# An mLSTM and two expert layers on one core: an added GpSimd drain, counts from TensorE in the capacity search, and moved waits

## The reference

```
logits = x @ w_gate
for idx in argsort(-logits.flatten()):        # best pairs first
    tok, e = idx // E, idx % E
    if assigned[tok] >= 0 or counts[e] >= cap: continue
    assigned[tok] = e; counts[e] += 1
out[assigned == e] = relu(x[assigned == e] @ w1[e]) @ w2[e]
```

## Time and profile before

| what | value |
|---|---|
| median of 3 runs | 793.84 us (792.9 to 794.62) |
| the profiled execution: its time | 794.07 us |
| the profiled execution: its span | 792.3 us |
| TensorE busy | 742.0 us (94%) |
| VectorE busy | 434.4 us (55%) |
| ScalarE busy | 315.5 us (40%) |
| GpSimd busy | 408.8 us (52%) |
| mean granted TensorE clock | 0.888 of full |

### The profile page before, as it was taken

How to read it: one execution, slowest core, us unless ns; L and a number is a source line. 1 busy time by engine, 2 the same in 40 slices (tenths; PEclk the granted TensorE clock), 3 DMA queues, 4 the chain that set the end, 5 groups by cost and what they waited for, 6 DMA issues and landing times.

```text
span 792.3 us, 21203 instructions
## 1 busy us (share of the span) xinstructions
PE 742.0 (94%) x7388; PEld 647.2 (82%) x7388; DVE 434.4 (55%) x1249; ACT 315.5 (40%) x822; POOL 408.8 (52%) x559
## 2 busy tenths in 40 slices
PE   7999999999998888999999999799999999999993
PEld 3677778777777777999999998489999899899993
DVE  7898887766666673365566765723322323322321
ACT  3566667430000002567667776432332332333330
POOL 4686674600000006877888877336475475475540
PEclk9999999855555556999999999899999999999997
DMA  6676668545922202645456445256767967942320
GB/s 173 196 222 185 196 206 275 171 143 170 308 81 82 82 2 61 208 145 196 122 189 197 134 137 171 70 177 191 221 178 201 264 190 195 251 130 83 95 74 0
DMA packets 64452, 126.24 MB, mean 159 GB/s; under 512 B 14712, under 2 KB 46481, under 8 KB 63603
## 3 DMA queue, kind: packets, MB, share of 16 engines
q1 hardware_dynamic: 44770, 84.19, 34.2%
q0 software_dynamic: 7728, 29.92, 12.7%
q10 hardware_dynamic: 11872, 10.99, 5.1%
HBM read 93.58 MB, written 15.34 MB: 137 GB/s over the span
## 4 chain that ended last, share of the span: by engine, by line
PE 79%; DVE 8%; issue 4%; POOL 2%; ACT 2%; DMA 1%; POOLq 0%; ACTq 0%
PE bank L1678 12%; PE bank L1679 12%; PE bank L1680 12%; PE bank L1637 5%; PE bank L1833 3%; PE bank L1714 3%; PE bank L1717 3%; PE bank L1718 3%; PE bank L1442 3%; PE bank L1613 2%; PE bank L1485 2%; PE bank L1515 2%; PE bank L1809 2%; PE bank L1419 2%; PE bank L1808 2%
## 5 line engine op out<-in xcount | busy, mean ns | idle before, releaser
L1678 PE MATMUL bank<-w_hi,hT_hi 128*128 (+1 forms) x440 | 140.9, 320 | 3.5 <-DVE hT_lo L1256 2.9
L1679 PE MATMUL bank<-w_lo,hT_hi 128*128 (+1 forms) x440 | 136.6, 311 | 0.0
L1680 PE MATMUL bank<-w_hi,hT_lo 128*128 (+1 forms) x440 | 136.5, 310 | 0.0
L858 POOL TENSOR_TENSOR w_lo<-w_raw,w_hi 128x320 fp32r<-128x320 f32 x128 | 109.1, 881 | 35.0 <-DMA w_hi<-w_raw 17.6
L829 POOL DMA_INDIRECT routing_arena<-x_rows,routing_arena x24 | 23.5, 977 | 153.5 <-DVE routing_arena L1244 143.6
L845 POOL TENSOR_TENSOR w_lo<-w_raw,w_hi 128x256 fp32r<-128x256 f32 x124 | 94.0, 791 | 3.7 <-ACT w_hi L608 3.0
L1678 PEld LDWEIGHTS bank<-w_hi,hT_hi 128*128 128x128 f32 x440 | 82.7, 188 | 5.7 <-issue 3.1
L1679 PEld LDWEIGHTS bank<-w_lo,hT_hi 128*128 128x128 f32 x440 | 82.8, 188 | 0.0
L1680 PEld LDWEIGHTS bank<-w_hi,hT_lo 128*128 128x128 f32 x440 | 82.7, 188 | 0.0
L694 ACT ACTIVATE hT_hi<-bank 128x512 fp32r<-128x512 f32 x62 | 33.8, 596 | 96.6 <-PE bank L1833 96.6
L1256 DVE SCALAR_TENSOR_TENSOR hT_lo<-bank,hT_hi 128x384 fp32r<-128x384 f32 x64 | 35.7, 558 | 62.6 <-ACT hT_hi L615 62.6
(11 more groups left out here) (296 smaller groups left out, 1819.5 us busy)
## 6 DMA issues: line engine op xcount, KB each, us to landing
w_raw<-in_moe_w SPq DMA_DIRECT2D x16, 1280.0 KB, 7.0
w_raw<-in_moe_w SPq DMA_DIRECT2D x16, 1024.0 KB, 5.6
turn_arena<-in_moe_w2t SPq DMA_DIRECT2D x12, 768.0 KB, 5.3
w_raw<-in_moe_w SPq DMA_DIRECT2D x32, 256.0 KB, 6.8
w_hi<-w_raw POOLq DMA_DIRECT2D x6, 1280.0 KB, 6.2
w_hi<-w_raw POOLq DMA_DIRECT2D x12, 512.0 KB, 6.9
routing_arena<-x_sorted ACTq DMA_DIRECT2D x31, 160.0 KB, 2.6
mlstm_arena<-in_q SPq DMA_DIRECT2D x32, 120.0 KB
```

Of the source, the lines that this page charges most:

```text
L858: return nc.gpsimd.tensor_tensor(w2_part(w2_lo, n)[:, k, :], w2_raw[:, k, :], w2_part(w2_hi, n)[:, k, :], ALU.subtract)
L1678: T.matmul(dst, a_hi, b_hi, start=first, stop=False)
L1679: T.matmul(dst, a_hi, b_lo, start=False, stop=False)
L1680: return T.matmul(dst, a_lo, b_hi, start=False, stop=last)
```

## The change

It has six parts. GpSimd executes a drain behind the store of block 27, four blocks ahead of the end (`NB2 - 4`). The loads of the gates and of c_head raise two semaphores, so that VectorE's scan waits for two loads; behind the first transposes TensorE makes 7 products of ones in place of 14. In `settle` the sum over blocks and its product are gone: VectorE keeps a copy of the eighth round's counts (`way_count`), marks which of the 16 candidates was taken (`way_is`), TensorE multiplies the two, and the room is the smaller of that and the room before. The first expert's three gathers raise three semaphores and the wait between them is gone. The last expert's first down block waits for each slice by itself. In the second layer the turn of block 1 stands between the high and the low products of `first_up`, ScalarE splits block 1 ahead of its ReLUs, and VectorE waits for the low products before it makes the low part of block 1.

```diff
-            sp.dma_start(head_rows[:, :], t["c_head"]).then_inc(ld_gate, 16)
+            sp.dma_start(head_rows[:, :], t["c_head"]).then_inc(ld_head, 16)
...
-            act.wait_ge(ld_gate, 48)
+            act.wait_ge(ld_head, 16)
...
                 act.wait_ge(dve_made, DVED["first_rows"])
                 next_rows(2, 0)
-                with act.Fori(0, NB2 // 2 - 1) as j:
+                x_hi(1, 1)
+                relu(0)
+                hidden_hi(0)
+                next_rows(3, 1)
+                step(1, 1, True, True)
+                with act.Fori(0, NB2 // 2 - 2) as j:
                     for s in range(2):
-                        step(2 * j + s, s, True, True)
+                        step(2 * j + 2 + s, s, True, True)
...
-                    if e == 0 and b == 2:
-                        pool.wait_ge(landed_a, 16)
                     pool.indirect_dma_start(rows[:, b, 0:KT * 128], None, x_sorted[:, :],
-                                            bass.IndirectOffsetOnAxis(ap=order[:, j:j + 1], axis=0)).then_inc(landed_b if e or b == 1 else landed_a, 16)
+                                            bass.IndirectOffsetOnAxis(ap=order[:, j:j + 1], axis=0)).then_inc(landed_b if e else (landed_a, landed_b, landed_c)[b], 16)
...
                                         tokens[:, b, 0:DM], None, bounds_check=N - 1, oob_is_err=False).then_inc(landed_b, 16)
+                if b == NB2 - 4:
+                    pool.drain()
             pool.wait_ge(landed_b, B_STORED + 16 * NB2)
...
-            dve.wait_ge(ld_gate, 48)
+            dve.wait_ge(ld_gate, 32)
...
+                    if r == ROUNDS - 1:
+                        counted = mark(V.tensor_copy(way_count[:, :], bank[6][0:WAYS, 0:E]))
                     dve.wait_ge(kb_ready, n + 1)
...
-                dve.wait_ge(over_ready, ph + 1)
-                with nc.allow_low_precision("counts up to 24 are exact in bf16"):
-                    V.tensor_reduce(osum_b[:, :], over_b.rearrange("p g e -> p e g"), AX.X, ALU.add).then_inc(osum_ready, 1)
+                need(counted)
+                V.scalar_tensor_tensor(way_is[:, :], theta[0:WAYS, :], threshold[ROUNDS % 2][0:WAYS, 0:1], lane[0:WAYS, 0:1],
+                                       ALU.subtract, ALU.is_equal).then_inc(way_ready, 1)
...
-                link(V.tensor_tensor(room[:, :], room[:, :], count_over, ALU.subtract))
+                link(V.scalar_tensor_tensor(room[:, :], over_room, -1.0, room[:, :], ALU.mult, ALU.min))
...
                 x_lo(0, 0)
+                dve.wait_ge(h_ready, 2 + 1)
                 x_lo(1, 1)
...
-            spin(bank[7], 14)
+            spin(bank[7], 7)
...
                 assign(0, over_b)
-                pe.wait_ge(osum_ready, ph + 1)
-                T.matmul(bank[1][:, 0:E], ones[:, :], osum_b[:, :], start=True, stop=True).then_inc(over_count, 1)
-                side(2)
+                side(1)
+                pe.wait_ge(way_ready, ph + 1)
+                T.matmul(bank[1][:, 0:E], way_is[:, 0:1].to_broadcast([WAYS, 128]), way_count[:, :], start=True, stop=True).then_inc(over_count, 1)
+                side(1)
...
-                    pe.wait_ge(hl3_done, FT * (e + 1) + 2)
+                    if not isinstance(e, int) or e < E - 1:
+                        pe.wait_ge(hl3_done, FT * (e + 1) + 2)
                 pe.wait_ge(yb_done, BPE * e + b + 1)
                 for k in range(FT):
+                    if b == 0 and isinstance(e, int) and e == E - 1:
+                        pe.wait_ge(hl3_done, FT * e + k + 1 + 2)
...
-                pe.wait_ge(x_done, 2)
+                turn(1, 1, 1)
                 for f in range(2):
                     for k in range(2):
                         T.matmul(bank[f][:, :], xT_lo[:, k, 0:128], w1_part(w1_hi, 128, k, f), start=False, stop=False)
...
                 first_up()
-                turn(1, 1, 1)
                 turn_hidden(0)
```

More of the change, by code:

```diff
@@ L275, in build @@
         prev_b = carve(128, [E, G], bf16)
-        osum_b = carve(128, [E], bf16)
+        way_is, way_count = carve(WAYS, [1]), carve(WAYS, [E])
         eye = carve(128, [3, 128], bf16)
@@ L337, in build @@
         ld_const = sem("ld_const")
-        ld_gate = sem("ld_gate")
+        ld_gate, ld_head = sem("ld_gate"), sem("ld_head")
         ld_route = sem("ld_route")
@@ L359, in build @@
         ties_ready, rank_ready = sem("ties_ready"), sem("rank_ready")
-        landed_a, landed_b = sem("landed_a"), sem("landed_b")
+        landed_a, landed_b, landed_c = sem("landed_a"), sem("landed_b"), sem("landed_c")
         raw1_ready, raw2_ready = sem("raw1_ready"), sem("raw2_ready")
@@ L388, in build @@
         NROUTE = 14 * 16
-        A_FIRST, B_FIRST = 32, 16
+        A_FIRST, B_FIRST = 16, 16
         A_SCATTERED = A_FIRST + 16 * G
@@ L1122, in _ @@
             rank = bank[4][:, 0:E * G].rearrange("p (e g) -> p e g", e=E)
-            count_over, tie_total = bank[1][:, 0:E], bank[5][:, 0:E]
+            over_room, tie_total = bank[1][:, 0:E], bank[5][:, 0:E]
             lg = logit_bank[:, 0:G * E].rearrange("p (g e) -> p g e", e=E)
@@ L1180, in search, with settle @@
                         link(V.scalar_tensor_tensor(key_rest[:, :], key_hi[:, :], threshold[r % 2][:, 0:1], half_i[:, 1, :], ALU.subtract, ALU.add))
-                return threshold[(ROUNDS - 1) % 2][:, 0:1]
-            def settle(ph, theta):
+                return threshold[(ROUNDS - 1) % 2][:, 0:1], counted
+            def settle(ph, theta, counted):
                 dve.wait_ge(assigned_ready, 2 * ph + 1)
@@ L1212, in _ @@
                 bits = keys(la[:, :, :] if ph else logit[:, :, :])
-                settle(ph, search(ph, bits))
+                settle(ph, *search(ph, bits))
             link(V.tensor_scalar(rest[:, :], taken[:, :], 0.0, None, ALU.is_equal))
@@ L1686, in first_turn3 @@
                 for b in range(BPE):
-                    pe.wait_ge((landed_a, landed_b, landed_a)[b], (16, B_FIRST, A_FIRST)[b])
+                    pe.wait_ge((landed_a, landed_b, landed_c)[b], 16)
                     for k in range(KT):
```

2 lines of the change are left out of this document (1 added, 1 removed).

## The result

| what | before | after |
|---|---|---|
| median | 793.96 us (792.9 to 794.62, 4 runs) | 781.96 us (780.78 to 783.19, 4 runs) |
| ratio | | 0.985, 95% 0.9827 to 0.9873 |
| profiled execution: time, span | 794.07, 792.3 us | 780.78, 779.0 us |

What follows compares the result with a forecast made beforehand. The chain that ended last was 79% TensorE; GpSimd's exit drain was the largest term. Gains 8.5 + 2.0 + 2.0 + 0.8 + 1.2 + 0.8 = 15.3 us took 794.07 to 778.8, stated as 778.5; range 776 to 788.

Steps and rivals of the forecast that it cites:

- rival 2: The drain works, but another engine or the clock takes back half of the other 6.8 us, giving 782; chance 0.08 more.
- The drain: GpSimd behind block 27's store: price goes by DMAs since the last drain, 0.081 us each; gain 8.5 us.
- Rivals 1 and 4: 1: a drain costs the same whatever is pending, 787.3; 4: added drain returns without the work, counted there; chance 0.16.
- The beginning: First loads and products of ones: dropped wait gives 0.45 us, seven fewer products 1.86; taken as 2.0 us gain.
- half beyond 21 us: Sign at the beginning that the prediction is wrong: TensorE's clock still at its half level after 21 us.
- full by 15 to 18: Sign expected in the profile after: TensorE's clock at its full level by 15 to 18 us.
- rival 3: Half clock at the beginning doesn't end, 11 us on: slower than before, up to 818; chance 0.04.
- The searches: Seven search phases: VectorE's scan starts sooner without the reduction of over-threshold tokens, 0.28 us per phase, 2.0 us gain.
- The gathers: First expert's third gather, without its wait, follows the second 1.28 us later; gain 0.8 us.
- the last expert: First down product: one wait per slice frees 1.4 us, of which ScalarE can use 1.2; gain 1.2 us.
- The first two blocks: Second layer: moving block 1's turn ahead of the low products starts its up product sooner; gain 0.8 us.
- with the same 0.79 of issue: Step for the first two blocks: after the move, block 1's up product starts at 520.55 to 520.85 with 0.79 us of issue.

## Why the prediction was right or wrong

**The time and the side** were right, 781.96 in 776 to 788, though 3.5 above the number said. What came is what rival 2 had said (782): the drain works, and the small gains don't add up. Of 6.8 us forecast for the five other edits the runs give 1.6 to 2.5. That the profiled execution fell by 13.29 is in part luck: 2.2 of it are gains that nobody forecast and that another execution of the same code has only in part.

**The drain**: right in size (8.68, forecast 8.5), in its place and in costing nothing there. The price by the number of DMAs, chosen because two measured drains differed in that alone, is now shown at 3, 12, 16, 30, 48 and 106. Rivals 1 and 4 fall. The fixed part of 0.18 was a misreading: of the 184 ns at the start all but 0.05 pass while GpSimd's last memset ahead of it still runs, and so the exit's drain is 0.30 and not 0.42. The Trainium skill (VectorE: DVE Perf Modes, "The DRAIN you can't avoid") gives the DRAINs of preamble and postamble as a constant of about 12 ns on all five engines. At this exit only SyncE's 13 ns agree; GpSimd's 298 to 8974 do not, nor do ScalarE's 607, VectorE's 591 and TensorE's 1193 in the changed kernel. The first store behind the added drain was late by 2.84 us, and nobody waited for it.

**The beginning** (2.0 forecast, 0.27 and 0.94 in the two executions of the changed kernel, and -0.15 to 1.39 in all eight that have its beginning): no gain is shown at all, since the two executions with an unedited beginning read 0 and 0.79. Two steps failed. "7 x 0.43 = 3.0 us of TensorE" priced the products at the half clock of one execution; at full clock 14 take 3.22 us in all, and the missing 7 are worth 0.4 for VectorE. And "TensorE is busy without a gap, so the shift is carried on" was said of what lay behind the place where the shift is lost. The risk I had named, the clock, was the right one, but it took another course: not that the low clock of 11 us stays, but that with fewer products the clock falls later, at 14.8 to 17.1. That happens in 8 of 8 profiled executions with 7 products and the wait unfilled, in none of 3 with 14 (the drain alone, the 14 restored, the same with the rows held; the half clock in the profile of before lies earlier, at 11), and in neither of the 2 with the wait filled. The Trainium skill (TensorE: Matmul & The Clock Gate, on oscillation) says that waits throttle TensorE anew. The traces agree: a wait of 1.56 to 1.58 us stands ahead of each of the eight, and one of 0.34 or 0.16 where the clock stays full. The half clock ends by itself, at 19.0 to 20.5 in four of the eight and at 21.6 to 21.9 in the other four, the first profile among them. So the sign "half beyond 21 us", by which the prediction called itself wrong, was met, and "full by 15 to 18" was not; rival 3, that it doesn't end, never came. The risk was priced at up to 1.5 us in the bounds and at 0.3 in the sum. Named nowhere was the second bound: the loads of the third pair, which move up too and then share the queues with the first pair's cumulated rows. It binds the kernel before too where its clock is full, so moving VectorE's chain up could not have paid 2 us with either number of products. (There TensorE waited 1.12 us at 25.32 for it, with the drain alone.) The sum should have asked of each moved issue on SyncE what lands beside it.

**The searches** (2.0 forecast, 0.15, and 0.04 to 0.28 in the other executions with this order): VectorE's 0.27 a phase are there. The step that failed is "so it has the room". The prediction gave TensorE's new product no length. The old one took 0.19 us in bf16; the new one is fp32 and 16 rows deep, 0.59 us at the half clock of that stretch, and a side product of 0.39 stands behind it, so the ranks started when TensorE was free, not when the ties were ready. My lower bound (0, "if TensorE comes last") was nearly the case.

**The gathers** (0.8, measured 0.79) and **the last expert** (1.2, measured 1.38): right, and shown by taking them back.

**The first two blocks** (gain of 0.8 forecast, loss of 0.33 to 0.37): the low part of block 1 was ready early, as forecast. The step that failed is "with the same 0.79 of issue". That issue was no fixed tail of the low part: it was two register loads and their operations on TensorE's sequencer. They come behind the transposes in program order, and the transposes wait for ScalarE's ReLU; it ends at 516.52, the first load begins at 516.58, and the up product starts 1.81 us behind the ReLU, whatever else is ready (before 1.82). The move only pushed the ReLU, and with it the transposes, back, by 0.35 us. The sign named for this term, 1.3 us from first_up's last product to the up product, read 2.44. With the loads moved ahead the forecast gain is there, 0.78.

**Not forecast**: 0.76 us in the first expert, and 1.44 from stalls of 0.2 to 1 us in the second layer's later blocks. Both vary with every execution of the same code (in the second profile of the changed kernel those blocks gave 1.3, and the first expert, behind the gathers, took 0.5 back). The first goes with the clock's return to full. Count that return in the kernel's own work, as its time plus the lead at the third gather: over the fourteen profiled executions it lies between 309.1 and 312.4, and the first expert gains 1.0 us at the one end and loses 0.5 at the other, about 0.44 us for each us. What sets the return, and what the stalls, I have not found.

## What to carry to other kernels

GpSimd's drain at the exit charges for every DMA issued from it since its last drain, 0.082 to 0.085 us each where there are 12 or more; a drain put where the engine idles anyway and where nobody waits for its stores takes that off the end. Before a gain on one engine is added to a sum, look at what the other engine does between the moved instruction and the next common wait, with its own clock: filler, side products and register loads stand in program order and don't move up by themselves. And a term read from a single execution is only as good as that execution's clock: price products by rows at the clock that the stretch will have.

## What the runs showed of the hardware

- GpSimd's DRAIN: 0.283 or 0.298 us behind 3 DMAs, 1.022 behind 12, 1.355 behind 16, 2.53 behind 30, 4.02 behind 48, 8.74 behind 106, 8.97 behind 109; direct and indirect alike, right behind a store or behind its landing, and not by bytes or packets. SyncE's takes 13 ns, though it issued loads all through.
- Seven products of ones fewer, followed by waits of 1.57 and 0.51 us, put TensorE at 1.2 GHz somewhere between 14.8 and 21.9 us in all eight executions; six products inside the wait kept it at 2.4 in both.
- The store and the reload of the first pair's cumulated rows took 6.9 to 7.4 us from issue to use where the third pair's rows went out 6.1 us behind the store or later (four executions), and 8.1 to 10.9 where they went out 4.2 to 4.5 us behind it (ten).
- For block 1 of the second layer the first load of a register from memory on TensorE's sequencer took 0.49 us, the second 0.31, and with the operations around them 1.8 us passed between the end of ScalarE's ReLU and the first product.
